# Reordering the opening of a fused attention and two-MLP kernel: six half blocks and three whole ones for the first tile's layer 1

## The reference

```python
def _attn_ref(q, k, v):            # 8 batches, 8 heads, 576 tokens, head 64
    k_p = k.reshape(B, H, Sp, pool, D).mean(axis=3)
    v_p = v.reshape(B, H, Sp, pool, D).mean(axis=3)
    scores = scale * np.matmul(q, k_p.transpose(0, 1, 3, 2))
    attn = softmax(scores)         # max subtracted, sum + 1e-9
    return np.matmul(attn, v_p)

def _moe_ref(x, w1, w2, w3, w_out):     # x: 4608 x 512, hidden 768
    h = np.maximum(np.maximum(x @ w1, x @ w2), x @ w3)
    return h @ w_out

def _moe2_ref(x, w_in, w_out):          # hidden 2048
    h = x @ w_in
    g = h - np.tanh(h)
    return g @ w_out
```

## Time and profile before

| | us |
|---|---|
| median of 3 runs | 1440.73 |
| lowest, highest | 1439.23, 1441.86 |
| the profiled execution's own time | 1439.83 |
| its span, first to last instruction | 1438.0 |
| PE busy | 1424.2 (99%) |
| DVE busy | 1006.7 (70%) |
| ACT busy | 653.8 (45%) |
| POOL busy | 96.4 (7%) |

### The profile page before, as it was taken

One profiled execution on the slowest core, in us unless ns is written; L12 is line 12 of the kernel. 1 busy time (PEld: TensorE's weight loads), 2 busy tenths in 40 slices (PEclk: granted clock), 3 DMA queues, 4 the chain that ended last, 5 costly groups with the idle time before them and its releaser, 6 DMA issues.

```text
span 1438.0 us, 26270 instructions
## 1 busy us (share of the span) xinstructions
PE 1424.2 (99%) x10794; PEld 1236.1 (86%) x10794; DVE 1006.7 (70%) x1765; ACT 653.8 (45%) x1291; POOL 96.4 (7%) x140
## 2 busy tenths in 40 slices
PE   8899999999999999999999999999999999999998
PEld 7888888888888878788899999999999999999997
DVE  7786666665656555534887777777777777777777
ACT  3322222222222221223676665666666566665655
POOL 2302121212121100000000000000000000000000
PEclk9999999999999999999999999999999999999999
DMA  6544444443534211155977666676766667676551
GB/s 224 200 148 138 167 142 166 143 165 127 180 128 152 99 60 60 52 198 208 326 271 256 220 234 228 214 254 219 254 220 225 235 218 256 213 250 223 194 184 52
DMA packets 81335, 269.74 MB, mean 188 GB/s; under 512 B 7168, under 2 KB 21504, under 8 KB 69568
## 3 DMA queue, kind: packets, MB, share of 16 engines
q1 hardware_dynamic: 81216, 268.07, 54.0%
HBM read 210.89 MB, written 57.15 MB: 186 GB/s over the span
## 4 chain that ended last, share of the span: by engine, by line
PE 95%; DVE 2%; DMA 2%; ACT 0%; issue 0%; SPq 0%; DVEq 0%; ACTq 0%
PE psum L676 29%; PE psum L716 27%; PE psum L740 25%; PE psum L690 10%; PE psum L619 2%; PE psum L659 2%; DMA v_first<-in_v 0%; DMA w_raw<-in_w 0%; DMA w_mid_raw<-in_w_mid 0%; DVE probs L1059 0%; DMA k_first<-in_k 0%; DMA k_raw<-in_k 0%; PE psum L803 0%; DVE h L1091 0%; PE psum L698 0%
## 5 line engine op out<-in xcount | busy, mean ns | idle before, releaser
L676 PE MATMUL psum<-x,w 128*128 128x512 f32 (+1 forms) x2160 | 452.7, 370 | 5.8 <-ACT first_copy L844 3.1
L676 PEld LDWEIGHTS psum<-x,w 128*128 128x128 f32 x2160 | 375.7, 188 | 77.1 <-ACT first_copy L844 3.3
L716 PE MATMUL psum<-w_out_s,g 128*128 128x512 f32 x1668 | 404.7, 391 | 0.5 <-DVE g L1126 0.4
L716 PEld LDWEIGHTS psum<-w_out_s,g 128*128 128x128 f32 x1668 | 304.3, 188 | 58.8 <-DVE g L1126 1.4
L740 PEld LDWEIGHTS psum<-x_even,ring 128*128 128x128 f32 x1680 | 212.7, 191 | 6.5
L740 PE MATMUL psum<-x_even,ring 128*128 128x256 f32 x1680 | 215.0, 283 | 0.0
L1131 DVE SCALAR_TENSOR_TENSOR poly<-poly,u_sq 128x512 f32<-128x512 f32 x144 | 99.0, 688 | 141.1 <-ACT poly L896 141.1
L740 PEld LDWEIGHTS psum<-x_odd,ring 128*128 128x128 f32 x1344 | 170.0, 191 | 5.0
L740 PE MATMUL psum<-x_odd,ring 128*128 128x256 f32 x1344 | 171.9, 283 | 0.0
L852 ACT ACTIVATE h<-best 128x512 fp32r<-128x512 f32 (+1 forms) x60 | 35.4, 589 | 276.1 <-DVE best L1085 276.1
L690 PE MATMUL psum<-h,w_mid_s 128*128 128x512 f32 x648 | 152.3, 391 | 0.0
(11 more groups left out here) (82 smaller groups left out, 1085.8 us busy)
## 6 DMA issues: line engine op xcount, KB each, us to landing
ring<-w_scratch SPq DMA_DIRECT2D x72, 1024.0 KB, 5.1
ring<-w_scratch SPq DMA_DIRECT2D x72, 768.0 KB, 4.4
x_scratch<-x_stage SPq DMA_DIRECT2D x18, 1024.0 KB, 4.2
x_odd<-x_scratch SPq DMA_DIRECT2D x28, 512.0 KB, 5.5
x_even<-x_scratch SPq DMA_DIRECT2D x28, 512.0 KB, 5.5
x_scratch<-x_stage SPq DMA_DIRECT2D x18, 768.0 KB, 3.4
w_scratch<-w_stage SPq DMA_DIRECT2D x32, 384.0 KB, 2.6
v_raw<-in_v SPq DMA_DIRECT2D x21, 512.0 KB, 4.6
```

The costliest lines, as they stand in the source:

```text
L676: mm = pe.matmul(psum[:, bank, 0:hi - lo], w123[:, m, ws, n, c, :], x[:, xs, c, lo:hi], start=(c == 0 and ws + xs == 0), stop=(c == KC1 - ...
L716: mm = pe.matmul(psum[:, j, :], g_of(c)[:, gs, j * P:(j + 1) * P], w_out_s[:, row_of(c), ws, :], start=(m == 0 and gs + ws == 0), stop=(m ...
```

## The change

The core of the diff. The list of the opening before layer 1, and of the first tile's layer 1:

```diff
-        ("warm", 14), ("score", 0), ("score", 1), ("exp", 0), ("exp", 1), ("warm", 14), ("pool_v",), ("warm", 9), ("norm", 0), ("turn", 0),
-        ("high", 0), ("norm", 1), ("turn", 1), ("low", 0), ("attend", 0), ("high", 1), ("low", 1), ("high", 2)]
+        ("warm", 14), ("score", 0), ("score", 1), ("shift", 0), ("shift", 1), ("exp", 0), ("exp", 1), ("warm", 14), ("pool_v",), ("warm", 6), ("norm", 0),
+        ("high", 0), ("norm", 1), ("turn", 1), ("turn", 0), ("first_low", 0), ("attend", 0), ("score", 2), ("score", 3),
+        ("first_low", 1), ("first_low", 2), ("high", 1), ("low", 1), ("high", 2), ("shift", 2)]
...
-    after_l1 = [[("high", 3), ("score", 2), ("score", 3), ("norm", 2), ("turn", 2)], [("high", 4), ("norm", 3)],
-                [("high", 5), ("turn", 3)], [], [("attend", 1)], [("high", 6)]]
-    for m in range(MC1):
-        if m == 1:
-            then(("l1", 0, m, 0, HALF), ("exp", 3), ("h1", 0, m, 0, HALF))
-        else:
-            l1(0, m, 0, HALF)
-        then(*after_l1[m])
-        if m > 1:
-            fill()
+    l1(0, 0, 0, HALF)
+    then(("high", 3), ("exp", 2), ("shift", 3), ("norm", 2), ("turn", 2))
+    then(("l1", 0, 1, 0, HALF), ("exp", 3), ("h1", 0, 1, 0, HALF), ("high", 4), ("norm", 3))
+    l1(0, 2, 0, HALF)
+    then(("turn", 3), ("attend", 1))
+    fill()
+    l1(0, 3, 0, TB)
+    fill()
+    then(("high", 5),)
+    l1(0, 4, 0, TB)
+    then(("score", 4), ("score", 5), ("norm", 4), ("turn", 4))
+    fill()
+    l1(0, 5, 0, TB)
+    then(("norm", 5), ("turn", 5))
+    fill()
+    l1(0, 0, HALF, TB)
+    then(("score", 6), ("score", 7), ("norm", 6), ("turn", 6), ("high", 6))
+    l1(0, 1, HALF, TB)
+    then(("norm", 7), ("turn", 7), ("high", 7))
+    l1(0, 2, HALF, TB)
+    fill()
```

The first normalization goes to POOL, the low part of piece 0 is made in three parts that the three products wait for one by one, and the first attend writes to banks 0 to 3 in place of 4 to 7, so that scores 2 and 3 (in banks 4 to 7) needn't wait for x:

```diff
+            pool.wait_ge(softmax_step, 3)
+            nc.gpsimd.tensor_tensor(probs[:, 0, :, 0:KEYS], probs[:, 0, :, 0:KEYS],
+                                    first_inv.unsqueeze(2).to_broadcast([P, GROUPS * 2, KEYS]), ALU.mult)\
+                .then_inc(first_normalized, 1)
...
+        def product_banks(n):
+
+            return 0 if n == 0 else 4
...
+            def first_piece_low(n):
+
+                _, raw, hi, lo = piece(0)
+                dve.wait_ge(piece_hi, 1)
+                nc.vector.tensor_tensor(lo[:, n], raw[:, n], as_f32(hi[:, n]), ALU.subtract).then_inc(first_low, 1)
```

And the loads on SP:

```diff
             load_q(3)
-            load_piece(3)
-
-            wait_filled(sp, ("l1", 0, 1, 0, HALF), NW - 1)
             for p in range(2):
                 load_k(1, p)
+            load_piece(3)
+
+            wait_filled(sp, ("l1", 0, 1, 0, HALF), NW - 1)
             load_piece(4)
-            load_piece(5)
-            for p in range(2):
-                load_v(1, p)
 
             for entry in ORDER:
-                if entry == ("l1", 0, 4, 0, HALF):
+                if entry == ("l1", 0, 3, 0, TB):
+                    load_piece(5)
+                    for p in range(2):
+                        load_v(1, p)
+                if entry == ("l1", 0, 5, 0, TB):
                     for i in range(MC1, MC1 + 2):
                         load_piece(i)
                     load_w_raw(0)
```

## The result

| | before | changed |
|---|---|---|
| median, us | 1440.84 (4 runs) | 1458.09 (4 runs) |
| lowest, highest | 1439.23, 1441.86 | 1457.08, 1458.72 |
| profiled execution: own time, span | 1439.83, 1438.0 | 1457.97, 1455.9 |
| ratio | | 1.0125, 95% interval 1.011 to 1.014 |

The change makes the kernel 17.3 us slower. The forecast was slower by 8.8, and the measured time lies above its range. Both new waits that it rests on are there; what it had wrong is what surrounds them. (One of the 11 executions of `opening_no_hold`, further down, took 2842.4 us at a granted clock of 1.00; nothing on record says why, and its ratio leaves it out.)

The account below looks back on a forecast made before the run. PE was taken to bound the kernel (95% of the last-ending chain). With both waits and tempo, layer 2 starts at 94.5 in place of 85.73: 1440.73 + 8.8 = 1449.5 us, range 1443 to 1454.

Parts of the forecast that it names:

- Both new waits: PE idle 7.7 us ahead of attend 1 for turn 3, and about 5 us ahead of layer 2 for POOL.
- shift at the end: Layer 2 starts 8.8 us later, and the end of the kernel moves by the same amount.
- the list of steps: From block 5's end to layer 2's start: maxima through POOL's two mid pieces, taking PE's start from 73.0 to 94.5.
- the 11.6 us of the strict rule: If DVE and POOL lock each other out fully, POOL loses up to 2.8 us and the sum is 11.6.
- Up to the end of the first block: nothing.: Opening through block 0: score 3 starts when q 3 lands at 21.0, block 0 ends at 26.4, gain 0.
- the wait ahead of attend 1: PE idle 7.7 us between block 2's end at 35.5 and attend 1 at 43.2, until turn 3 is over.
- queued behind high 4, which waits for the transfer of piece 4: ACT's copy of block 2's first product, needed for turn 3, waits for piece 4, landing at 36.0 after 5.0 us.
- Tempo after that idle time: PE runs slower after the idle time ahead of attend 1, costing 1.0 us, bounds 0 and 1.4.
- Behind it: After layer 2's start: moved k and v reductions cost nothing, otherwise one or two of 0.75 to 1.2 us.
- the faster mechanism (C): Rival: PE's saved work decides, layer 2 starts at 79.5, 6.2 us sooner, time 1434.5; chance 0.07.

Follow-up runs that it names:

- opening_no_hold: Kernel before with the changed opening, q 3 loaded ahead of piece 1 and piece 4 right behind piece 3: 1441.0 us, ratio 0.9999.
- quiet_queue: Changed kernel with q 3 loaded ahead of pieces 1 and 2, and pieces 1 to 3 and k held until block 0 filled its first bank: 1460.7 us.
- Opening_only: Changed kernel with blocks, high parts and loads of pieces 5 to 7 and of v in the order of before: 1439.8 us, ratio 0.999.
- blocks_only: Kernel before with the new block order alone, its opening as before: 1458.8 us, ratio 1.0117.
- fill_idle: Changed kernel with matmuls on ones, whose result nobody reads, put into PE's three idle times: 1453.1 us, ratio 1.0093.
- turn3_first: Changed kernel with exp 3, norm 3 and turn 3 moved ahead of block 1's copy and maxima: 1452.0 us, ratio 1.0075.
- mid_early: Changed kernel with both halves of w_mid made earlier (transfers one block sooner, high 6 behind block 5): 1454.6 us, ratio 1.0102.

## Why the prediction was wrong, point by point

The stations of the sum beside what was measured, in us of the span:

| | forecast | measured | off by, in this step |
|---|---|---|---|
| block 2's first half over | 35.5 | 39.6 | +4.1 |
| attend 1 starts | 43.2 | 45.9 | -1.4 |
| first whole block starts | 45.8 | 49.8 | +1.3 |
| block 5 over | 73.0 | 78.4 | +1.4 |
| layer 2 starts | 94.5 | 99.8 | -0.1 |
| shift at the end | 8.8 | 17.9 | +3.8 |

- **Right: what would bound, and where.** Both waits stand where they were put, with the releasers that were named. Layer 2's start is the best hit, and no luck, as each step of the list came out within 0.2 us: from the end of block 5 the list of steps (maxima, norm, turn, reduction, shifts, exponential, high part, two pieces on POOL) gave 21.5 us, 21.4 were measured. Of the lock between DVE and POOL the trace shows three ops of DVE stretched (to 0.77, 0.47 and 1.53 us) while POOL took 8.16 in all against 8.23 in the sum, so the 11.6 us of the strict rule were not called for.
- **Wrong: "Up to the end of the first block: nothing."** Block 0 was over at 29.8, not 26.4. The step that failed is that score 3 would start when q 3 landed: q 3 landed at 21.0 as forecast, but PE stood until 22.9, and for these 1.9 us, an "issue" gap, the prediction has no term: quiet_queue shows that it goes with the density of the transfers, and it ends 1.6 us behind a packet of the instruction queue. Another 1.2 us is half clock in block 0 (5.75 against 4.54), behind a standstill of 3.2 us. Opening_only shows why I would have been nearly right for the old blocks, where 3 us of lateness are free. With DVE's bank (1.0 us ahead of block 2's last product) this makes about the 4.1.
- **Right in size, in part by luck: the wait ahead of attend 1.** The load took 4.6 us (5.0 forecast), and from its landing at 38.7 to the end of turn 3 it was 7.1 (7.2 forecast). But the step "queued behind high 4, which waits for the transfer of piece 4" sets attend 1 by itself in blocks_only alone, where the wait is 10.7 us. In the changed kernel ACT came to high 4 at 38.8, as the load landed, and with the load sooner the wait stays 6.3. The sum lacks a second chain of the same length: from block 0 through shift 3, norm 2, turn 2 and block 1's maxima to high 4. Norm 2 and turn 2 stand nowhere in the sum up to attend 1. At the length that the list for layer 2 gives such a pair they would be 2.9 us; beside POOL the trace has 37.50 - 32.67 = 4.8. That this chain was no longer than the load was luck. The -1.4 in the table is block 2's later end (1.0, the bank) and the shorter load (0.4).
- **Mis-sized: "Tempo after that idle time", 1.0 us with bounds 0 and 1.4.** It measured 1.3 in attend 1 and 2.25 in the first whole block, and I priced it at one of three places only: block 0 had 1.2, layer 2's first pair 2.7 (11.0 in the chain against 8.2). That is some 7.5 us in all, of which the forecast held 1.0, and of which fill_idle won back 5.0 by the medians. Two mistakes: I took the price from 28 short matmuls at the start of the span, as an upper end, though nothing said that the stretch behind a gap would be no longer than that one; and I asked for it only where I saw the longest gap, not behind each. The Trainium skill's rule (TensorE: Matmul & The Clock Gate, "The HAM clock gate"), that PE slows when it has been idle and needs sustained work to come back, agrees with the granted clock of these rows at all three; I had cited it and then applied it once.
- **Missing: the turn of the banks.** Nine uses fewer turn every later use, by three steps on or one back, and the projection opens on a bank just filled: about 1.1 us, 600 us behind the change. "Behind it" named the fills only, and these did cost nothing.

The sum of the misses is 5.3 up to layer 2, 2.8 in it and 1.0 behind it: 9.1, the difference of 17.9 and 8.8. The forecast's direction, and that fewer matmul columns bought nothing, held: the faster mechanism (C) needed both waits away, and easing either in an experiment (turn3_first, mid_early) still left 11 to 15 us of loss. Both at once was not run.

## What to carry to other kernels

An idle time of PE costs its length and then a slow stretch behind it: price both, and at each gap, not only at the longest. When blocks are reordered, walk each other engine's queue from the last common point and take its ops at the length that they have beside their neighbour, since the order, not the amount of work, decided the wait ahead of attend 1 and at least part of the one ahead of layer 2. And a lateness that costs nothing today is covered by some wait: the same opening was free under the 3 us wait of the kernel before and cost about 4 us when that wait was removed.

## What I had not expected of the hardware

- The clock's fall behind about 3 us of standing is not certain: with 3.1 us it stayed at 1.00, with 3.0 it went to 0.50 for some 6 us in a kernel whose work up to there was the same. The length of the gap alone doesn't decide: in blocks_only the clock fell behind 2.3 us (0.50 from 90 to 92) and not behind 2.6 us ahead of layer 2. Some of the scatter of the kernel before (1437.6 to 1443.3 over all batches) may be this.
- PE can stand 2.9 us with every operand ready while the transfers run at a share of 1.07, and 0.45 us at the same place when they are at 0.03. Each such "issue" gap ended 1.2 to 1.6 us behind a 16 KB packet of the instruction queue, which came later when the loads were dense.
